# Routing tokens in four groups inside the delta-rule stage, with fixed row bases for the experts

## The reference

```python
# 1. delta rule, per batch b and head h (k_n is k divided by its norm)
for t in range(S):
    y[:, :, t] = einsum('bhd,bhde->bhe', q[:, :, t], state)
    v_old = einsum('bhde,bhd->bhe', state, kt)
    state = state + bt * einsum('bhd,bhe->bhde', kt, vt - v_old)
# 2. sticky top-1 mixture of 8 experts, hidden width 1024
for b in range(B):
    prev_e = -1
    for s in range(S):
        fresh_e = argmax(logits[b, s])
        e = fresh_e if s == 0 or local_gate[b, s] < 0.5 else prev_e
        prev_e = e
        p = softmax(logits[b, s])
        out[b, s] = p[e] * (relu(x[b, s] @ w1[e]) @ w2[e])
# 3. gated convolution, hidden width 1024, kernel 3
h = relu(x @ w_in)
gate = sigmoid(conv3(h, conv_w))
out = (h * gate) @ w_out
```

## Time and profile before

| stretch (us of the trace) | what runs | length |
|---|---|---|
| 0 to 167.9 | delta rule, with logits | 167.9 |
| 168 to 209.5 | router block | 41.5 |
| 209.5 to 214.82 | first rows loaded, turned and split | 5.3 |
| 214.82 to 228.40 | first tile, until the first `down` | 13.6 |
| 228.40 to 400.9 | the other tiles | 172.5 |
| to 529.1 | gather, gated convolution | 128.2 |

### The profile page before, as it was taken

How to read it: one execution, slowest core, us unless ns; L and a number is a source line. 1 busy time by engine, 2 the same in 40 slices (tenths; PEclk the granted TensorE clock), 3 DMA queues, 4 the chain that set the end, 5 groups by cost and what they waited for, 6 DMA issues and landing times.

```text
span 529.1 us, 15064 instructions
## 1 busy us (share of the span) xinstructions
PE 459.2 (87%) x6069; PEld 406.0 (77%) x6069; DVE 367.6 (69%) x557; ACT 287.8 (54%) x463; POOL 91.8 (17%) x130
## 2 busy tenths in 40 slices
PE   7889899979996200799999999999987799999997
PEld 4657888858784200689999899998986689999997
DVE  5997785842222670499999999999961467789661
ACT  4424444322333420599998998989950353444542
POOL 5516402030000185000100101001003500000000
PEclk9989999967999555699999999999999599999999
DMA  9563310270002453826854764641002400000202
GB/s 137 108 122 63 64 32 8 57 262 4 4 5 65 175 189 116 290 71 230 282 189 153 267 211 150 234 149 59 15 31 65 129 0 2 0 2 0 90 1 90
DMA packets 60826, 54.53 MB, mean 103 GB/s; under 512 B 41155, under 2 KB 54339, under 8 KB 60774
## 3 DMA queue, kind: packets, MB, share of 16 engines
q1 hardware_dynamic: 54694, 41.18, 26.7%
q0 software_dynamic: 3968, 12.19, 6.7%
q10 hardware_dynamic: 2112, 0.39, 0.5%
HBM read 76.16 MB, written 12.19 MB: 167 GB/s over the span
## 4 chain that ended last, share of the span: by engine, by line
PE 53%; issue 2%; DVE 2%; DMA 1%; ACT 1%; POOL 0%; DVEq 0%; POOLq 0%; ACTq 0%
PE ps L1758 5%; PE ps L1760 5%; PE ps L1759 5%; PE ps L1775 5%; PE ps L1776 5%; PE ps L1777 5%; PE ps L2029 3%; PE ps L2030 3%; PE ps L2031 3%; PE ps L2042 3%; PE ps L2043 3%; PE ps L2044 3%; PE ps L1767 3%; PE ps L1748 1%; PE ps L2017 1%
## 5 line engine op out<-in xcount | busy, mean ns | idle before, releaser
L1716 DVE TENSOR_TENSOR w2l<-raw,w2h 128x768 fp32r<-128x768 f32 x76 | 67.8, 953 | 6.8 <-ACT w2h L1659 6.6
L1716 DVE TENSOR_TENSOR w1l<-raw,w1h 128x1024 fp32r<-128x1024 f32 x54 | 62.9, 1219 | 3.4 <-ACT w1h L1659 1.4
L1659 ACT CAST w2h<-raw 128x768 fp32r<-128x768 f32 x76 | 58.2, 852 | 1.0 <-DMA raw<-in_moe_w_dram 1.0
L1659 ACT CAST w1h<-raw 128x1024 fp32r<-128x1024 f32 x54 | 53.6, 1069 | 1.0 <-DMA raw<-in_moe_w_dram 1.0
L1775 PE MATMUL ps<-w2h,hh 128*128 128x384 f32 x152 | 52.3, 344 | 1.8 <-DVE hl L1721 1.8
L1777 PE MATMUL ps<-w2h,hl 128*128 128x384 f32 x152 | 50.9, 335 | 0.0
L1776 PE MATMUL ps<-w2l,hh 128*128 128x384 f32 x152 | 50.8, 334 | 0.0
L1758 PE MATMUL ps<-w1h,xh 128*128 128x512 f32 x114 | 47.5, 417 | 1.6 <-DVE xl L1708 1.6
L1760 PE MATMUL ps<-w1h,xl 128*128 128x512 f32 x114 | 45.8, 401 | 0.0
L1759 PE MATMUL ps<-w1l,xh 128*128 128x512 f32 x114 | 45.3, 398 | 0.0
L855 PE MATMUL ps<-idle_b 128*128 128x512 bf16 (+3 forms) x130 | 36.9, 388 | 1.8 <-DVE idle_b L627 1.8
(11 more groups left out here) (221 smaller groups left out, 1044.6 us busy)
## 6 DMA issues: line engine op xcount, KB each, us to landing
raw<-in_moe_w_dram SPq DMA_DIRECT2D x57, 512.0 KB
raw<-in_moe_w_dram SPq DMA_DIRECT2D x76, 384.0 KB
x_sorted<-x_all SPq DMA_DIRECT2D x1, 3648.0 KB, 12.8
x_all<-x_sorted POOLq DMA_DIRECT2D x19, 192.0 KB, 2.8
y_sorted<-x_all POOLq DMA_DIRECT2D x19, 192.0 KB, 2.2
q_nat<-in_q_dram SPq DMA_DIRECT2D x24, 96.0 KB, 3.2
v_nat<-in_v_dram SPq DMA_DIRECT2D x24, 96.0 KB, 3.2
out_dram<-res SPq DMA_DIRECT2D x12, 192.0 KB, 2.4
```

Source lines behind the costliest of these rows:

```text
L1659: act.copy(hi(par), raw).then_inc(s_wh, 1)
L1716: dve.tensor_tensor(lo(par), raw, hi(par).bitcast(F32), ALU.subtract).then_inc(s_wl, 1)
```

## The change

The router block is gone. Its work is part of the delta-rule block, in the groups of steps 0 to 3, 4 to 7, 8 to 10, and 11. Each expert's rows now begin at a fixed base (expert number times 1,664), so a group's tokens have their places as soon as the group is ranked, with the rank of the group before as the scan's start. Experts' rows are 8 wide (not batch by expert, 16), with the two batches one behind the other in the columns. `route_tokens`, `route_sequence`, `route_rank` and `route_rows` are called in VectorE's list between the steps' operations; PE gets `route_rows`, `route_back` and `route_tiles`, ACT `route_keep`. POOL issues `scatter(n)` at the end of its list in the delta-rule block, then the load of the first tile's rows. A table `tile_row` says where a tile's rows are, and every tile's load reads it. Every expert has at least one tile, so the first expert is number 0, and its weights are loaded within the delta-rule stage, into the buffers that held keys, queries and one of the masks. The zero fill shrinks from 19 x 128 rows to 7 x 128; in its stead 8 copies of 128 zero rows (`pad`) go behind the last row of each expert, two in the delta-rule block and six in SP's list of the experts' block.

The split of the first expert's `w1` is now at the start of the experts' block. The loads and splits of `w_in` and `w_out` are at the end of it, in four halves; the probabilities (13 VectorE operations) stand ahead of the last tile's `hidden`. The products of the convolution wait for the halves. PE gets `warm(10)` and `warm(5)` around the first tile's transposition. The lists of all engines in the delta-rule block are in another order from near the start on.

```diff
@@ build_program
-    x_sorted = nc.dram_tensor("x_sorted", [NT * P, DM], F32, kind="Internal").ap()
+    CAP = B * S + P
+    x_sorted = nc.dram_tensor("x_sorted", [E * CAP + (E - 1) * P, DM], F32, kind="Internal").ap()
...
+        def pad(sp, e):
+
+            r = sp.value_load(pad_row[0:1, e:e + 1], min_val=0, max_val=E * CAP)
+            sp.dma_start(x_sorted[bass.ds(r, P), :], x_sorted[E * CAP:E * CAP + P, :]).then_inc(s_pads[min(e, 2)], 16)
...
@@ attention, SP
-            sp.dma_start(x_sorted.rearrange("(n p) d -> p n d", p=P),
-                         x_all[:, NSTEP - 1].unsqueeze(1).to_broadcast([P, NT, DM])).then_inc(s_zero, 16)
+            sp.dma_start(x_sorted[E * CAP:].rearrange("(n p) d -> p n d", p=P),
+                         x_all[:, NSTEP - 1].unsqueeze(1).to_broadcast([P, E - 1, DM])).then_inc(s_zero, 16)
             sp.wait_ge(s_zero, 16)
+            sp.wait_ge(s_tk, NSTEP)
+            sp.wait_ge(s_sq, NG)
+            sp.wait_ge(s_kb, NG)
+            for c in range(CD):
+                dst, src = weight_load(c, 0)
+                sp.dma_start(dst, src).then_inc(s_raw[c], 16)
+            sp.wait_ge(s_tq, NSTEP)
+            sp.wait_ge(s_z32, 3)
+            for c in range(CD, NC):
+                dst, src = weight_load(c, 0)
+                sp.dma_start(dst, src).then_inc(s_raw[c], 16)
+            sp.wait_ge(s_rd, routed(NGR - 1, "pad_row"))
+            pad(sp, 0)
+            pad(sp, 1)
@@ attention, POOL
+            def scatter(n):
+                p = [a <= n < z for a, z in GROUPS].index(True)
+                if n == GROUPS[p][0]:
+                    pool.wait_ge(s_rd, routed(p, "token rows"))
+                    pool.wait_ge(s_x, GROUPS[p][1])
+                pool.indirect_dma_start(out=x_sorted, out_offset=bass.IndirectOffsetOnAxis(pos_i[:, n:n + 1], 0),
+                                        in_=x_all[:, n, :], in_offset=None).then_inc(s_sc, 16)
...
+            scatter(11)
+            pool.wait_ge(s_sc, 16 * NSTEP)
+            pool.wait_ge(s_pads[0], 16)
+            x_load(pool, 0, 0, slice(0, P))
@@ attention, ACT
+            def route_keep(p):
+                act.wait_ge(s_kv, 2 * p + 1)
+                if p:
+                    act.wait_ge(s_rd, routed(p - 1, "sequence 1"))
+                w = P * (GROUPS[p][1] - GROUPS[p][0])
+                act.copy(keep[:, 0:w], bank[BK][0:E, 0:w]).then_inc(s_keep, 1)
@@ attention, VectorE
+            def route_sequence(p):
+                m = GROUPS[p][1] - GROUPS[p][0]
+                dve.wait_ge(s_kv, 2 * p + 2)
+                dve.wait_ge(s_keep, p + 1)
+                for b in range(B):
...
+                    step(p, f"sequence {b}", dve.tensor_tensor_scan(e_seq[p % 2][:, c], keep[:, c], bank[BQ][0:E, c], before,
+                                                                    ALU.mult, ALU.add))
+                need(p, "sequence 1")
+                step(p, "one hot", dve.tensor_scalar(one_hot[:, 0:m * P], e_seq[p % 2][:, 0:m * P], tables.row_e[:, 0:1], None,
+                                                     ALU.is_equal))
...
+            def route_rows(p):
+                a, z = GROUPS[p]
+                dve.wait_ge(s_pp, p + 1)
+                step(p, "token rows", dve.tensor_scalar(pos_i[:, a:z], bank[BK][:, 0:z - a], -1.0, None, ALU.add))
...
@@ attention, PE
+            def route_rows(p):
+                a, z = GROUPS[p]
+                m = z - a
+                pe.wait_ge(s_rd, routed(p, "kv rows"))
+                if p == 0:
+                    pe.wait_ge(s_gq, NSTEP)
+                for k in range(2):
+                    o = bank[BK + k][0:E, 0:m * P].rearrange("e (b n t) -> e b n t", b=B, n=m)
+                    for i in range(m):
+                        r = pe.matmul(o[:, :, i], kvr[:, k, a + i], tables.ident_b[:].rearrange("p (b t) -> p b t", b=B),
+                                      start=True, stop=True)
+                    r.then_inc(s_kv, 1)
...
+            route_rows(2)
+            w_mul(11)
+            warm(9, 2, s_lg, 3)
+            out_mul(11)
...
@@ experts, SP
             for c in W1C:
                 load(c, e1, c + 1, new1)
+            for e in range(2, E):
+                pad(sp, e)
+            sp.dma_start(cw_r, conv_w).then_inc(s_cw, 16)
...
+            sp.wait_ge(s_wl, w1_split(NT - 1))
+            sp.dma_start(raw1[:], w_in.rearrange("(c p) f -> p c f", p=P)).then_inc(s_cwt[0], 16)
+            sp.wait_ge(s_wl, NT * NC)
+            sp.dma_start(raw2[:], w_out.rearrange("(c p) d -> p c d", p=P)).then_inc(s_cwt[1], 16)
@@ experts, POOL
-            x_load(pool, 0, 0)
+            pool.wait_ge(s_pads[1], 16)
             x_load(pool, 1, 1)
+            pool.wait_ge(s_pads[2], 16 * (E - 2))
             rows_in(0, 0)
@@ experts, ACT
+            weights(0, 0, W1C)
             rows(0, 0)
...
             hidden(NT - 1)
+            conv_weight(0)
+            conv_weight(1)
+            conv_weight(2)
             result(NT - 1, 0, 16 * ((NT - 1) // 2))
+            conv_weight(3)
@@ experts, VectorE
             weights(w2_split(NT - 2), 0, W2C)
+            probabilities()
             hidden(NT - 1)
+            for i in range(len(halves)):
+                conv_weight(i)
@@ experts, PE
+            warm(10)
             rows(0, 0, 16)
+            warm(5)
             up(0, 0, first=True)
```

1043 lines of the change are left out of this document (556 added, 487 removed).

## The result

Nine runs of the changed kernel gave a median of 526.63 us (522.9 to 529.37), nine of the kernel before 533.47 us (528.79 to 551.49). The ratio is 0.988, with a 95% interval of 0.984 to 0.993: 1.2% faster, where I had forecast 501 us and a range from 490 to 515. The sign was right, the size was not: 6 to 7 us came of 33. The profiled execution took 524.4 us, with a span of 522.9.

A forecast was written before the change was run, and what follows sets the result against it. The router block was read as a 49.9 us stretch where PE, which bounds the other stages, stands still. 529.1 - 32.5 (A) - 2.9 (B) + 0 (C) + 6.0 (D) = 499.7 us, plus 1.5 outside: 501, range 490 to 515.

The forecast's parts named there:

- Term B: Delta rule up to the last output copy: burst, order and inside routing together -2.9 us.
- The burst: Delta rule: zero fill delays PE's instructions and lowers the clock, price 9.2 us; half saved, -4.6, bounds 0 and -9.2.
- The sign that I had named for a wrong forecast: End of the delta rule: a last output copy after 170 us would show the forecast wrong.
- Rival 2: Delta rule: the burst costs twice, a stall and half clock in each load part, +4.6 + 9.2, 515 us; chance 0.15.
- hidden on POOL: Delta rule: the scatters of groups 0 to 2 are hidden on POOL, which was idle for 70.6 us there.
- Order and routing inside: Delta rule: earlier masks remove two VectorE waits, -4.5 us; routing between the steps adds +6.2 us.
- Term A: Last output copy to first expert product: one group left to route, 49.9 us becomes 17.4, -32.5 us.
- Term C: First tile: idle products may raise the clock, the third tile's rows may come late; 0, bounds -2.7 and +4 us.
- Term D: Last tile and behind: probability operations delay the last low part, clock may fall; +6.0 us, bounds +3 and +9.
- Rival 1: Delta rule: the burst harms nothing now, 495 us, or 490 with a kept clock in the last tile; chance 0.20.
- rival 4: Delta rule: DMA load from 100 to 155 us brings repeated stalls of 9.2 us each, slower than before; chance 0.03.

The follow-up runs named there:

- a_end2: Kernel of `a_best2` with all seven weight loads behind the delta rule's last right side, repeated as a control: ratio 0.941, median 502.7 us.
- a_best2: Changed kernel, zero fill in three pieces, weight loads spread over steps, third tile's rows waiting for one zero copy, probabilities behind last low part: ratio 0.945, median 503.1 us.
- a_again: The changed kernel, unedited, as a control on another chip: ratio 0.994, median 529.2 us.
- a_pads: Changed kernel, with the third tile's rows waiting for one zero copy alone, issued first: ratio 0.951, median 517.5 us.
- b_paced: Kernel before the change, with its zero fill cut into seven pieces that wait for outputs of steps 5 to 10: ratio 0.983.
- a_end_r: Kernel of `a_best2` with both weight loads and scatters behind the delta rule's last right side: ratio 0.941, median 508.5 us.
- a_end: Kernel of `a_best2` with all seven weight loads behind the delta rule's last right side: ratio 0.934, median 503.6 us.

## Why the prediction was wrong, point by point

- **Term B, "The burst", is the step that failed.** I wrote: "I take half the price as saved, -4.6, bounds 0 and -9.2". The mechanism was read rightly from the earlier trace rows: a burst, a stall, a fall of the clock. The size was not. I had taken the price of one execution, with its 13.7 us of half clock, as the most that the burst costs, and that length is nothing fixed: 34 us in the changed kernel, 3.4 to 47.8 in the others. From the fifth output copy to the tenth the changed kernel took 65.0 us; with the clock kept the same list takes 48.6 (`a_end2`) to 49.9 (`a_best2`). The stall, the half clock and what the first scatters did in it cost 15 to 16.5 us, where I had 4.6 left in the sum. The sign that I had named for a wrong forecast, a last copy after 170 us, came: 180.3.
- **Rival 2 came nearest.** It charged the burst with twice 9.2 us, 18.4, for "a stall and half clock in each part". The profiled execution of the changed kernel had one stall and one long half clock instead (`a_again` and `a_pads` had two stalls), at 15 to 16.5 us. Its 515 was still short, by the scatters (next point) and by terms A and C. I gave it 0.15.
- **The scatters beside PE were "hidden on POOL".** POOL was idle, that was right, but in the profiled execution PE fell to a few products per 0.73 us beside them: 4.4 to 5.4 us in the last two steps (18.0 from the tenth copy to the twelfth, against 13.6 in `a_best2` and 12.6 in `a_end2`). My sum had nothing for it. I had bounded the routing by its operations on VectorE and PE, and not by what its transfers do to PE's instructions. That the scatters cause it is argued from their coincidence, not shown: the versions that move them ran only where the pattern did not appear.
- **Order and routing inside.** -4.5 + 6.2 = +1.7 came out near: with the clock kept, 61.2 and 63.5 us from the fifth copy on, against 59.5 for the old list (`b_paced`), +1.7 to +4. The profiles are of several chips, and the -4.5 was not measured apart. The last step took 9.3 us against 5.2 (+4.1; I had +5.2).
- **Term A**, -32.5, came as -30.2. The last scatter ended 7.3 us behind the copy (7.6 forecast), the first load was issued at 10.6 (11.2). The step missed is the joint behind it: I set the split of `w1` at the load, but it stands behind the barrier. Timeline of the changed kernel:

```profile
190.89 0.58 POOL L103 DMA_DIRECT2D x_all<-x_sorted  x1 [3.30 <-DMA x_sorted<-x_sorted]
...
194.39 2.94 ACT L1756 CAST w1h<-raw 128x1024 fp32r<-128x1024 f32 x3 [8.84 <-PEq L166]
...
199.98 0.50 PE L1901 MATMUL ps<-w1h,xh 128*128 128x512 f32 x1
```

  From 194.39 to the product it is 5.6 us, as summed; the 3.5 us from the start of the load's issue to there were not in the sum.
- **Term C** came as +3.6, within its bounds (+4), and is made of two parts. PE waited 6.15 us for the third tile's rows, where I had 2 to 4: the six zero copies took SP 6.96 us, 1.16 each and not 0.6. The rest of the tile gained 2.5 us, near the bound of 2.7. Of this the two warm calls account for 1.7 (12.7 us without them, 11.1 with), and they cost 0.5 ahead of it.
- **Term D** came as +5.5 for +6.0, in part by luck. The 13 operations took 1.8 us (385.53 to 387.30), not 3.3, since each one starts before the last one's duration is over; PE's gap was 2.92 us, not 4.6: +1.4 for +3.0. The fall of the clock came and took 1.6 us (6.0 against 4.4), for 2.2. Behind it 0.5 us were added, for 0.8. The missing 2.0 us stand where I had left everything as it is: from the first `down` to the second it took 11.6 us, against 9.5 before.
- **Slips in the prediction's sums.** The terms' bounds add up to 484 and 523, not 487 and 520. Rival 1 with a kept clock in D comes to 493, by D's own 2.2 us, not 490. In rival 4 the fifth stall is enough for 2% slower, not the sixth. The measured 526.6 lies outside either way.

With the clock kept the time comes near the sum, by terms that offset each other. `a_best2`'s profiled execution took 501.8 us, but it has edits for C and D that the forecast did not have. Its terms are B -1.5, A -30.2, C -2.5, D +7.1 and -1.6 at the end. My estimate for the changed kernel itself, from `a_best2`'s 163.4 us up to the last copy and the changed kernel's own stages behind it, is 507.5 us: inside the range, 6 above the forecast.

## What to carry to other kernels

A transfer can have a price even where nothing waits for its data. Here long stalls of PE for its instructions stood beside bulk DMAs and dense runs of small products, and the fall of the clock behind a stall could cost several times the stall. Spreading the transfers, or putting them where PE does not set the time, gave 503 to 516 us and 503 to 504 us as medians; the intervals of the two do not tell them apart. Look at the granted clock by slices before trusting a sum of durations. When a cost shows in one profiled execution, its length is a sample: bound it by the whole stretch that the clock could stay down, not by the one seen.

## What the runs showed of the hardware

- PE stood for its instructions at places that lie multiples of 256 instructions apart, and went on 1.2 to 1.5 us behind the end of a 16,384-byte packet on the instruction queue (all eighteen stalls of 1.14 to 3.49 us). Without transfers near, such gaps were 0.5 to 0.9 us.
- Half clock behind a stall lasted from 3.4 to 47.8 us. PE was busy for 92% and more of it, mostly with products of 32 to 48 columns, in all profiles but that of the kernel before (85%, part of the stall inside). What brings the clock back was not settled.
- Half clock cost some 0.4 us per us in these stretches. From the 7th copy to the 10th `a_end_r` (23.9 us of it), `a_end` (27.3) and `a_pads` (34.1) took 9.9, 11.3 and 15.5 us more than `a_end2`, with their stalls of 1.40, 1.40 and 2.75 us in it (0.55 in `a_end2`).
- Scatters of 192 KB, issued every 1.27 us, went with five or so products of PE per 0.73 us in four profiles, three of them from one chip, and in none of the nine from three other chips that had scatters beside the same call.
- The 12 scatters of the changed kernel took 0.95 to 1.20 us each, none the 7.41 us of the earlier trace rows. No large operation of two inputs in SBUF ran beside their start, so which of the two readings of that row is right stays open.
